# The last scatter on its own semaphore, awaited by SyncE, and an extra GpSimd drain

## What is computed

```python
attn_out = _attn_ref(q, k, v)                 # causal window of 64, B=4, H=8, S=576, D=64
x = attn_out.transpose(0, 2, 1, 3).reshape(2304, 512)
x = ((x @ w1) * (x @ w2)) @ w3 @ w_out        # w1, w2: 512x1024; w3: 1024x1024; w_out: 1024x512
logits = x @ w_gate                           # 8 experts, each token goes to its argmax
out[mask] = gate_w * eom * (relu(x[mask] @ ew1[e]) @ ew2[e])   # per expert e; 512 -> 1024 -> 512
```

## Time and profile before

| | us |
|---|---|
| median of 3 runs | 739.81 (739.04 to 739.93) |
| the profiled execution | 740.34 |
| its span, first to last instruction | 738.5 |
| PE busy | 709.2 (96% of the span) |
| POOL busy | 119.5 (16%) |

### The profile page before, as it was taken

How to read it: one execution, slowest core, us unless ns; L and a number is a source line. 1 busy time by engine, 2 the same in 40 slices (tenths; PEclk the granted TensorE clock), 3 DMA queues, 4 the chain that set the end, 5 groups by cost and what they waited for, 6 DMA issues and landing times.

```text
span 738.5 us, 15143 instructions
## 1 busy us (share of the span) xinstructions
PE 709.2 (96%) x5136; PEld 645.4 (87%) x5137; DVE 330.4 (45%) x666; ACT 297.6 (40%) x720; POOL 119.5 (16%) x191
## 2 busy tenths in 40 slices
PE   5999999999999999999999998999999999999994
PEld 4889999999999989999999997778888888888883
DVE  3477554512135424552420368755456554652210
ACT  3477454522135534453211253344446444642211
POOL 5012011100011111111001001112222222222111
PEclk9999999999999999999999999999999999999998
DMA  9586111320012241201043034466265744411110
GB/s 295 178 307 222 53 48 54 102 86 1 15 51 65 59 129 38 79 23 43 1 154 132 1 103 150 151 212 227 78 222 187 235 155 156 151 36 40 38 37 29
DMA packets 48063, 80.14 MB, mean 109 GB/s; under 512 B 5325, under 2 KB 29901, under 8 KB 48016
## 3 DMA queue, kind: packets, MB, share of 16 engines
q1 hardware_dynamic: 42976, 64.01, 26.8%
q0 software_dynamic: 5040, 15.47, 6.0%
HBM read 70.03 MB, written 10.49 MB: 109 GB/s over the span
## 4 chain that ended last, share of the span: by engine, by line
PE 90%; DVE 4%; DMA 2%; ACT 2%; issue 1%; POOL 0%; SPq 0%; DVEq 0%; POOLq 0%; ACTq 0%
PE bank L450 26%; PE bank L452 25%; PE bank L451 25%; PE bank L524 3%; PE bank L648 2%; PE bank L502 2%; PE bank L514 2%; DMA w3r<-in_w3T 2%; DVE wbuf L962 1%; PE bank L626 1%; PE bank L611 1%; PE bank L462 1%; PE bank L488 0%; PE bank L484 0%; DVE w3l L900 0%
## 5 line engine op out<-in xcount | busy, mean ns | idle before, releaser
L450 PE MATMUL bank<-Wh,abh 128*128 128x272 f32 (+1 forms) x288 | 84.0, 292 | 0.0
L452 PE MATMUL bank<-Wh,abl 128*128 128x272 f32 (+1 forms) x288 | 82.1, 285 | 0.0
L451 PE MATMUL bank<-Wl,abh 128*128 128x272 f32 (+1 forms) x288 | 81.8, 284 | 0.0
L962 DVE TENSOR_TENSOR wbuf<-raw,wbuf 128x1024 f32 (+1 forms) x64 | 75.4, 1221 | 12.3 <-ACT wbuf L770 11.6
L705 ACT ACTIVATE prob<-prob,nmx 128x128 f32<-128x128 f32 x144 | 56.3, 392 | 60.7 <-DVE nmx L879 60.7
L1257 POOL TENSOR_TENSOR prob<-prob,rec 128x384 f32<-128x384 f32 x48 | 39.7, 828 | 214.0 <-DVE rec L889 210.2
L1126 DVE TENSOR_TENSOR hTl<-bank,hTh 128x512 fp32r<-128x512 f32 x44 | 28.4, 686 | 96.4 <-ACT hTh L807 96.0
L450 PE MATMUL bank<-wbuf,hTh 128*128 (+1 forms) x176 | 70.6, 401 | 0.7 <-DVE hTl L1126 0.6
L450 PE MATMUL bank<-wbuf,xsTh 128*128 (+1 forms) x176 | 70.3, 400 | 0.6 <-DVE xsTl L1001 0.6
L452 PE MATMUL bank<-wbuf,hTl 128*128 (+1 forms) x176 | 68.8, 391 | 0.0
L452 PE MATMUL bank<-wbuf,xsTl 128*128 (+1 forms) x176 | 68.6, 390 | 0.0
(11 more groups left out here) (200 smaller groups left out, 1494.4 us busy)
## 6 DMA issues: line engine op xcount, KB each, us to landing
raw<-in_expert_w SPq DMA_DIRECT2D x64, 512.0 KB, 4.6
qT<-in_qT SPq DMA_DIRECT2D x24, 192.0 KB, 2.9
kT<-in_kT SPq DMA_DIRECT2D x24, 192.0 KB, 3.4
x_rows<-x_sb POOLq DMA_DIRECT2D x18, 256.0 KB, 2.3
w3r<-in_w3T SPq DMA_DIRECT2D x8, 512.0 KB, 3.9
wo<-in_w_out SPq DMA_DIRECT2D x8, 256.0 KB, 7.3
woT<-in_w_outT SPq DMA_DIRECT2D x4, 512.0 KB, 7.4
vA<-in_v SPq DMA_DIRECT2D x16, 128.0 KB, 2.2
```

Of the source, the lines that this page charges most:

```text
L450: pe.matmul(dst, lh, rh, start=first, stop=False)
L451: pe.matmul(dst, lh, rl, start=False, stop=False)
L452: return pe.matmul(dst, ll, rh, start=False, stop=last)
L962: dve.tensor_tensor(wbuf[:, bass.ds(wcol(e, part, 1, c * PC), PC)], raw[part * NP1 + c][:, :], f32(wbuf[:, bass.ds(wcol(e, part, 0, c * PC ...
```

## The change

1. Two semaphores are added, `y_last` and `y_last_out`.
2. ACT's scaling of the last slot (tail 2) raises `y_last` in place of `y_ok`. Its waits and its work are the same.
3. GpSimd's scatter of the last slot waits for `xs_in` and then `y_last`, and signals its landing on `y_last_out` in place of `y_out`. GpSimd no longer waits for that landing, and doesn't raise `y_free` after it.
4. SP waits, at the end of its program, for `y_last_out` to reach 16.
5. GpSimd executes a drain at the start of its body for tail 1.

```diff
@@ -440,6 +441,7 @@
                 for c in range(2 * NP1):
                     sp.wait_ge(ew_lo[c // NP1], e * NP1 + (c % NP1 + 1 - NP1))
                     load_piece(e, c)
+            sp.wait_ge(y_last_out, 16)
...
-            def y_scaled(s, last=0):
+            def y_scaled(s):
                 act.wait_ge(y_done, s + 2)
                 act.wait_ge(y_free, s + 1)
-                act.activation(y_sb[:, :], bank[5 + last][:, :], ACT.Copy, scale=ssc[:, bass.ds(s, 1)]).then_inc(y_ok, 1)
+                act.activation(y_sb[:, :], bank[5][:, :], ACT.Copy, scale=ssc[:, bass.ds(s, 1)]).then_inc(y_ok, 1)
 
             def body(s, tail=0):
                 if tail == 2:
-                    return y_scaled(s, 1)
+                    act.wait_ge(y_done, s + 2)
+                    act.wait_ge(y_free, s + 1)
+                    act.activation(y_sb[:, :], bank[6][:, :], ACT.Copy, scale=ssc[:, bass.ds(s, 1)]).then_inc(y_last, 1)
+                    return
...
-            def scatter(s):
-                pool.wait_ge(y_ok, s + 2)
+            def scatter(out_ok):
                 pool.sem_inc(turn, 1)
                 pool.indirect_dma_start(out=out, out_offset=bass.IndirectOffsetOnAxis(ap=sidc[:, 0:1], axis=0),
-                                        in_=y_sb[:, :], in_offset=None, bounds_check=last_row, oob_is_err=False).then_inc(y_out, 16)
-                pool.wait_ge(y_out, s * 16 + 16)
-                pool.sem_inc(y_free, 1)
+                                        in_=y_sb[:, :], in_offset=None, bounds_check=last_row, oob_is_err=False).then_inc(out_ok, 16)
...
             def body(s, tail=0):
+                if tail == 1:
+                    pool.drain()
                 pool.tensor_copy(sidc[:, 0:1], sid[:, bass.ds(s, 1)]).then_inc(pool_c, 1)
...
-                scatter(s)
                 if tail == 2:
                     pool.wait_ge(xs_in, s * 16 + 32)
+                    pool.wait_ge(y_last, 1)
+                    scatter(y_last_out)
+                else:
+                    pool.wait_ge(y_ok, s + 2)
+                    scatter(y_out)
+                    pool.wait_ge(y_out, s * 16 + 16)
+                    pool.sem_inc(y_free, 1)
```

More of the change, by code:

```diff
@@ L229, in build @@
         y_done, y_ok, y_out, y_free, turn = sem("y_done"), sem("y_ok"), sem("y_out"), sem("y_free"), sem("turn")
+        y_last, y_last_out = sem("y_last"), sem("y_last_out")
         f32 = lambda ap: ap.bitcast(F32)
```

## The result

| | before | after |
|---|---|---|
| median | 739.87 us (6 runs, 739.04 to 741.25) | 734.56 us (6 runs, 733.73 to 735.70) |
| ratio | | 0.9925, 95% interval 0.9912 to 0.9939 |
| profiled execution | 740.34 us | 734.87 us |
| its span | 738.5 us | 733.2 us |

The median fell by 5.3 us, 0.7%, as forecast (734.5). Run again beside other kernels, the changed kernel had 734.41 us against 740.18, ratio 0.9926 (0.9913 to 0.9938).

A forecast was written before the change was run, and what follows sets the result against it. TensorE, busy 96%, bounds the kernel; its exit is serial on GpSimd. SP's arrival 733.0 + barrier 0.2 gives span 733.2, 5.3 us under 738.5; from median 739.81, 734.5 us. Range 733.6 to 738.0, about 0.86.

The forecast's parts named there:

- What the drain's time is made of: GpSimd's last drain at the exit: its 5.22 us read as 0.18 plus 0.080 for each of 63 transfers.
- a price per transfer: In GpSimd's drains: each transfer issued since the last drain costs 0.080 us, estimated from two points.
- The price besides: Part of a GpSimd drain that is not per transfer: 0.18 us, from the drain at the program's start.
- The argument by the empty stretch: At the exit, 5.5 us without engine work or DMA traffic: the drain's 5.22 us are its own.
- The added drain: At tail 1, from 716.6: 5.1 us for 61 transfers, hidden in GpSimd's idle time, 0 on the path.
- Its cover: Slack at tail 1: the added drain may take 5.1 + 1.3 + 0.8 = 7.2 us before the end moves.
- the sum: Part-by-part timing to the exit: SP's arrival 733.0 + 0.2 = 733.2, or GpSimd's drain, if it waits, 733.3.
- The rival of a stretched drain: At tail 1, the drain stretches beside others' work and loses its cover: 745.2 us at 3.5 times; chance 0.05.
- The removed wait: At the exit: last drain covers 2 transfers, 0.34 us, ending at 731.4, or by 733.1 if it waits for landing.
- SP and the barrier: At the exit: SP sees the landing at 732.8, arrives by 733.0, and the barrier adds 0.2 us.
- The rivals of a fixed price: Last drain again takes 5.22 us: started earlier, 737.8 us, chance 0.06; after the landing, 739.5 us, chance 0.07.
- A late notice: At the exit, the queue retires its last transfer some 5.5 us after landing: no change, within that case's 0.07.

The follow-up runs named there:

- experiments 6: The kernel before with 18 more tiny GpSimd transfers to a spare tensor, three at the end of each chunk: 741.83 us (one run).
- experiment 7: The changed kernel with a further GpSimd drain at the end of each of the six chunks: 735.00 us (one run).
- experiment 8: The changed kernel with three drains in a row at tail 1 in place of one: 735.35 us (one run).
- Experiment 9: The changed kernel with 48 more tiny GpSimd transfers, eight at the end of each chunk: 736.61 us (one run).
- experiment 4: The changed kernel without SP's wait for the last landing: 733.40 us (4 runs), ratio 0.9915.
- experiment 2: The changed kernel without its added drain, so with the semaphores alone: 738.20 us (10 runs), ratio 0.9980.
- experiment 1: The kernel before with the added drain at tail 1 alone: 735.15 us (5 runs), ratio 0.9933.

## Why the prediction held

*What the drain's time is made of.* The step on which everything hung was the reading of two rows, 0.18 us before any transfer and 5.22 behind 63, as a price per transfer. It held: 0.082 us measured, 0.080 taken. The price besides was mis-sized: 0.18 taken, with four memsets among it, and 0.04 found; for 61 transfers the two errors cancel, since both prices go through the same 5.22 us for 63. The forecast had two points, which any law fits, and an argument; the result alone, with 5.06 us for 61, fits a price per transfer, and that it is one was shown by the experiments. The argument by the empty stretch was right too, in that nothing was waited for. What only one step of it suggested, experiments 6, 7 and 8 showed: each transfer counts alike, and only once.

*The added drain.* Forecast 5.1 us from 716.6, ready for `y_ok` at 722.5; it took 5.06, and the scatter behind it didn't move. Its cover was put at 7.2 us. Experiment 9 held GpSimd for 9.0 us and lost 1.3 to 1.4 us, so the cover is about 7.6. Two things make it more than 7.2. `y_free` was taken as raised with the copy at 727.66, and in the changed kernel L1324 raises it at 727.4, 0.2 us earlier. And the copy follows the drain's end by 0.5 us in the changed kernel (721.7 to 722.20), as the sum had it, but by 0.15 in experiment 9 (725.96 to 726.11); why, no run shows. The rival of a stretched drain had 0.05; 0.209 us in 18 of 20 loop drains beside a busy VectorE, and 5.057 in five profiles of four kernels, speak against it; the most that any drain here was stretched is 0.03 us (experiment 7). The copies of the earlier trace rows that took up to five times their least were no measure for a drain.

*The removed wait.* Left open was whether the last drain waits for the scatter in flight. It ends with the landing, also without SP's wait (experiment 4), later than the 731.4 of a drain that doesn't wait; the sum allowed up to 0.34 us behind the landing, and it was 0.1. The Trainium skill says that a drain waits for its engine to be fully idle (PSUM — Partial Sum Buffer, section Engine vs sequencer instructions). By the instructions in the trace this doesn't account for the end here: the scatter's was over at 731.0 in the changed kernel and the drain ended at 732.9, with the landing. The drain is recorded from 729.8, not from 731.06 as the rivals had it, but its end is as if it did no work until the scatter's instruction was done (experiment 2), which comes to the same time. That the drain and SP's path end within 0.1 us of each other is what made 733.2 right whichever came last: the forecast of the time didn't hang on the open question.

*SP and the barrier.* SP's arrival was put at 733.0 and the barrier at 0.2 us; its drain stands at 732.9 and the span ends at 733.2. If the drain waits for the landing by itself, SP's wait is a second guard; if it only takes a fixed time, SP's wait is the one that holds the end for a slower landing. Its cost was forecast, by the sum, as nothing over the landing, and experiment 4 finds 0.1 us or less.

*The rivals of a fixed price.* Both fell: experiment 1 has a last drain of 0.22 us, experiment 8 one of 0.03. A late notice would have kept the drain of experiment 1 long, and fell with them. The Trainium skill's constant drain of about 12 ns on every engine (VectorE: DVE Perf Modes, section The DRAIN you can't avoid) is that of the runtime's code around a kernel, and the exit here is the framework's. SP's 7 ns in every run are near it; of GpSimd's drains the least is 34 ns and the longest 8977.

*The shares.* The forecast counted 5.3 us as one sum. By part, the added drain alone is worth 4.9 and the semaphores, once it is there, 0.4 (the semaphores alone 2.0, and the drain, once they are there, 3.3): the wait that they remove from GpSimd, 731.0 to 732.8, is spent in the last drain instead, and what is saved is the drain's own 0.22 us and the step from wait to drain.

## What to carry to other kernels

When a span ends in microseconds without any engine at work, read the exit's own line: the drain there can be as long as two dozen matmuls of 0.23 us, and it is in no busy time. GpSimd's drain pays for every transfer that it has issued since its last drain, so a kernel with many of them can pay on the way, at a place where GpSimd is idle for longer than count times price, and not at a place where the next transfer is already late. Count the transfers before moving a drain, and split the change into its parts: here one added instruction carried nearly all of it.

## What was not expected of the hardware

- The price goes by the transfer, 0.082 us each for a 256 KB gather and for a store of 16 rows of 32 bytes, from 1 to 109 transfers without a bend.
- GpSimd's last drain ends 0.1 us after the landing of its open transfer, with or without SP's wait; whether it waits for the landing or takes a fixed time is not shown.
- Two drains with no transfer before them took 0.169 and 0.034 us; the difference isn't explained by any run here.
- TensorE's granted clock averages 0.66 and 0.71 over 465 to 470 us in the changed kernel's two profiles and 0.68 in the second of the kernel with a drain at every slot, and 1.00 in the first of that kernel, in that without SP's wait and in that of the kernel before. There the kernel passes from the dense stage to the experts, and TensorE had pauses around it (busy 17.7 of the 20 us from 455 to 475 in the kernel before, which kept its clock). The kernel with a drain at every slot shows both, so it can differ between executions of one program; it is a part of the few us by which single spans differ.
